# Other span widths in a gated recurrence with a feed-forward layer: 512, 512 and 496 pairs in place of 480, 512 and 512

## The reference, cut to what matters

```python
sig = 1.0 / (1.0 + np.exp(-f_logit))                 # (2, 6080, 256)
f = lower_bound + (1.0 - lower_bound) * sig
for t in range(S):
    h = f[:, t] * h + (1.0 - f[:, t]) * x[:, t]
    y[:, t] = h
h = y.reshape(B * S, D) @ w_in                       # (12160, 256) @ (256, 2048)
g = np.where(h >= 1, h, np.where(h <= -1, 0.0, (h + 1) ** 2 / 4))
return g @ w_out                                     # (12160, 2048) @ (2048, 256)
```

## Time and profile before

| what | us |
| --- | --- |
| median of 3 runs (992.54 to 993.21) | 992.62 |
| the profiled execution | 992.79 |
| its span, first to last instruction | 990.9 |
| TensorE busy | 985.0 (99%) |
| ScalarE busy | 873.6 (88%) |
| VectorE busy | 865.9 (87%) |
| GpSimd busy | 0.2 |
| the chain that ended last | 99% on TensorE |
| granted TensorE clock | 1.00 in all slices |
| DMA | 42.37 MB, 43 GB/s in the mean |

### The profile page before, as it was taken

How to read it: one execution, slowest core, us unless ns; L and a number is a source line. 1 busy time by engine, 2 the same in 40 slices (tenths; PEclk the granted TensorE clock), 3 DMA queues, 4 the chain that set the end, 5 groups by cost and what they waited for, 6 DMA issues and landing times.

```text
span 990.9 us, 12871 instructions
## 1 busy us (share of the span) xinstructions
PE 985.0 (99%) x4366; PEld 817.4 (82%) x4366; DVE 865.9 (87%) x1305; ACT 873.6 (88%) x1543; POOL 0.2 (0%) x4
## 2 busy tenths in 40 slices
PE   9999999999999999999999999999999999999998
PEld 6888888888888888888888888888888888888887
DVE  7998988988988888898888989889888889898775
ACT  8898989989988988998998898899898899898886
POOL 0000000000000000000000000000000000000000
PEclk9999999999999999999999999999999999999999
DMA  7202102101200210210120120021021012000101
GB/s 231 104 1 86 41 1 86 43 1 43 86 1 1 85 43 1 85 43 1 44 85 1 25 88 17 1 83 43 1 83 46 0 42 83 1 1 1 43 1 41
DMA packets 14577, 42.37 MB, mean 43 GB/s; under 512 B 1584, under 2 KB 4912, under 8 KB 14512
## 3 DMA queue, kind: packets, MB, share of 16 engines
q1 hardware_dynamic: 14224, 41.30, 12.2%
q10 hardware_dynamic: 288, 0.26, 0.1%
HBM read 29.10 MB, written 12.45 MB: 42 GB/s over the span
## 4 chain that ended last, share of the span: by engine, by line
PE 99%; DMA 0%; SPq 0%; ACT 0%; issue 0%
PE acc L942 18%; PE acc L943 18%; PE acc L944 18%; PE chain L942 9%; PE chain L943 9%; PE chain L944 9%; PE cross L943 4%; PE cross L942 4%; PE cross L944 4%; PE side L943 2%; PE side L944 2%; PE side L942 2%; DMA w_in_near<-w_in_pairs 0%; PE chain L1103 0%; PE side L1103 0%; PE cross L1103 0%
## 5 line engine op out<-in xcount | busy, mean ns | idle before, releaser
L942 PE MATMUL acc<-g_hi,w_out_lo 128*128 128x512 f32 (+2 forms) x768 | 297.7, 388 | 0.0
L943 PE MATMUL acc<-g_lo,w_out_hi 128*128 128x512 f32 (+2 forms) x768 | 297.3, 387 | 0.0
L944 PE MATMUL acc<-g_hi,w_out_hi 128*128 128x512 f32 (+2 forms) x768 | 297.3, 387 | 0.0
L405 ACT CAST g_hi<-g 128x512 fp32r<-128x512 f32 (+2 forms) x384 | 236.3, 615 | 41.2 <-DVE g L736 35.5
L751 DVE TENSOR_TENSOR g_lo<-g,g_hi 128x512 fp32r<-128x512 f32 (+2 forms) x384 | 262.2, 683 | 9.1 <-ACT g_hi L405 0.5
L398 ACT ACTIVATE g<-g 128x512 f32<-128x512 f32 (+2 forms) x384 | 240.9, 628 | 3.7
L736 DVE SCALAR_TENSOR_TENSOR g<-g,h 128x512 f32<-128x512 f32 (+1 forms) x264 | 180.9, 685 | 46.0 <-ACT g L398 42.7
L380 ACT ACTIVATE g<-h 128x512 f32<-128x512 f32 (+1 forms) x264 | 163.2, 632 | 26.9 <-DVE h L711 24.5
L942 PEld LDWEIGHTS acc<-g_hi,w_out_lo 128*128 128x128 f32 x768 | 144.1, 188 | 30.3 <-DVE g_lo L751 1.2
L944 PEld LDWEIGHTS acc<-g_hi,w_out_hi 128*128 128x128 f32 x768 | 144.2, 188 | 28.5
L943 PEld LDWEIGHTS acc<-g_lo,w_out_hi 128*128 128x128 f32 x768 | 144.2, 188 | 28.2
(11 more groups left out here) (91 smaller groups left out, 955.8 us busy)
## 6 DMA issues: line engine op xcount, KB each, us to landing
gate<-f_logit_chunks SPq DMA_DIRECT2D x18, 512.0 KB, 4.0
y<-x_chunks SPq DMA_DIRECT2D x18, 512.0 KB, 4.0
out_chunks<-result SPq DMA_DIRECT2D x9, 1024.0 KB, 4.2
w_out_f<-w_out_pairs SPq DMA_DIRECT2D x8, 256.0 KB, 4.9
y<-x_chunks SPq DMA_DIRECT2D x4, 496.0 KB, 4.0
gate<-f_logit_chunks SPq DMA_DIRECT2D x4, 496.0 KB, 4.1
w_in_near<-w_in_pairs SPq DMA_DIRECT2D x10, 128.0 KB, 4.4
out_chunks<-result SPq DMA_DIRECT2D x1, 992.0 KB, 4.2
```

Source lines behind the costliest of these rows:

```text
L405: nc.scalar.copy(g_hi[:, t, 0:cols], g[:, t, 0:cols]).then_inc(g_hi_ready[t], 1)
L942: nc.tensor.matmul(dst, w_lo, v_hi, start=start, stop=False, skip_group_check=more)
L943: nc.tensor.matmul(dst, w_hi, v_lo, start=False, stop=False, skip_group_check=more)
L944: return nc.tensor.matmul(dst, w_hi, v_hi, start=False, stop=stop, skip_group_check=more)
```

## The change

Span 0 gets 512 pairs like its neighbours. To keep 3040 pairs in batch 0, spans 8 and 10 get 496 in place of 512. Batch 1 is as before (spans 9 and 11 have 496). All tiles, loads, matmuls and operations follow from `width(q)`.

```diff
-FULL, FIRST_SHORT, LAST_SHORT = 512, 480, 496
+FULL, SHORT = 512, 496
@@
 def width(q):
-    if q == 0:
-        return FIRST_SHORT
-    return LAST_SHORT if q in (SPANS - 1 - BATCH, SPANS - 1) else FULL
+    return SHORT if q >= SPANS - 2 * BATCH else FULL
```

## The result

The changed kernel takes 994.99 us (median of 14 runs, 994.34 to 995.46), the kernel before 992.80 beside it (14 runs): ratio 1.0022, 95% interval 1.0015 to 1.0029. It is slower by 2.2 us, where 991.2 was forecast with a range up to 992.8. The profiled execution has a span of 992.8 us against 990.9.

What follows compares the result with a forecast made beforehand. TensorE, busy 99%, was taken to bound the kernel: matmuls times their step, plus opening and stalls. Terms 3.60 - 4.80 + 0.62 - 0.45 - 0.10 - 0.27 = -1.40 us gave 991.2 from 992.62, range 990.7 to 992.8.

Steps and rivals of the forecast that it cites:

- Preparing the next span: 496-wide windows preparing 496-wide spans (8, 9, 10) stall 0.02 us three times, against 0.32 before: -0.27 us.
- Rival A: First span stays 40 cycles above its columns, so its 512-wide matmuls take 230.0 ns: +1.20 us, 992.4; chance 0.18.
- Rival B: Stalls while preparing the next span stay full, three times 0.32 us: 0.91 above the forecast sum, 992.1; chance 0.14.
- Rival C: First span's 512-wide matmuls hold 236.7 ns because engines and weight loads use memory densely: +3.6 us, 994.8; chance 0.03.
- all cases beyond 2 us slower: Whole kernel slower by over 0.2%, mainly through 236.7 ns matmuls in the first span; chance 0.04.
- 360 x 10.0 = +3.60 for the first span: First span's 360 matmuls go from 480 to 512 columns, 216.7 to 226.7 ns each: +3.60 us.
- -4.80 for spans 8 and 10: 720 matmuls in these spans go from 512 to 496 columns, 226.7 to 220.0 ns each: -4.80 us.
- The stalls of window 3: First span's weight loads waiting for VectorE's g_lo: 0.45 of 0.65 us disappears behind longer matmuls, -0.45 us.
- The 0.22 in window 2: Time lost at the window's start, where the weight load waits for VectorE's g_lo: 13.22 us for 13.00 due.
- the change of spans: At 88 to 106 us, where 480 and 512 columns mix, mixing costs could go: -0.10 us, bounds -0.20 and 0.
- The opening: Before TensorE streams: larger half-loads +0.22, VectorE's drives and scans +0.29, last raw group +0.11; together +0.62 us.

Runs made afterwards that it cites:

- the first experiment: Changed kernel with ScalarE copying u3 ahead of the split of the next span's T1, T2 in windows j = 6: 990.93 us against 992.67, ratio 0.9985.

## Why the prediction was wrong

**The step that failed** is "Preparing the next span". I had found the event, counted that the weight load of p4 would come 0.12 us after its due time, and booked the stall of the one matmul behind it, 0.02 us, three times. It came 0.06 late (the copy ended 2.42 us after the start of p7, not 2.48), and its window lost 0.03 us, once. What I left out is what the late load does to all later matmuls: 25 windows x 0.15. The term was -0.27 and is -0.32 + 3.78 = +3.46. The number was in the trace of before: window 79 ran 0.15 us long over all its 45 matmuls, and I called it the wake of the stall and gave it the length of one window, because in that kernel 512-wide matmuls happened to follow.

**Rival A** held the right state, the offset of 40 cycles in place of 32, and I put it only on the first span. There it did not act, since 512 columns find back by themselves: windows 4 to 6 last 10.88. It would have, had the first span become 496 (10.72 in place of 10.56). I never asked of it what it does to the widths that the change makes more frequent. **Rival B** had three full stalls at 0.91 us; its place was right and its price counted by event, not by what follows. **Rival C** did not occur in the steady windows. Its price was read from rounded times: the three steps from 90.27 to 90.98 are 704 ns together, 234.7 each and not 236.7. The same 233 to 236 ns are seen where 512 columns mix with 480 in window 65 of the version with 480 in span 8, with no DMA transfer beside them. Whether the other engines' work has a part in it was not tested. I gave all cases beyond 2 us slower 0.04; that is where it ended.

**The surer terms.** 360 x 10.0 = +3.60 for the first span is right: 10.88 - 10.40 = 0.48 a window. The slope of 13.3 ns that the Trainium skill gives (TensorE: Matmul & The Clock Gate, Back-to-back issue gap) did not show in the first span, where the measured difference is 10.0; the 480 end of it sits 8 cycles high at both places where it was measured. -4.80 for spans 8 and 10 is right without the late load: 9.90 in the first experiment. The stalls of window 3 went from 0.65 to 11.07 - 10.88 = 0.19, which is -0.46 against -0.45, and the waits of the weight load for g_lo from 1.2 us to this row of the waits of after:

```profile
PEld acc L940 <- DVE g_lo L749: 0.2, 1, 0.2
```

The 0.22 in window 2 stayed (13.82 us for 60 x 0.2267 = 13.60). In the change of spans window 8 still takes 7.09, now for 30 x 226.7 = 6.80, so 0.12 of its excess went; window 9's went from 0.09 to 0.04 (10.17 and 10.24, for 10.08 and 10.20 due). Together that is -0.17 against -0.10.

**The opening** is a small miss. From the first raw matmul to the first 512-wide product it takes 7.85 us against 7.46, +0.39 for my 0.29 + 0.11. But the first raw matmul did not come 0.22 later; it starts at 6.79 here, and at 6.96, 7.29, 6.70, 7.05, 7.11 and 7.04 in the experiments with 512 in the first span, against 7.03 and 6.94 with 480. What 64 KB more ahead of the first weight block cost can't be seen in that spread; nearest to it is nothing. The 7.85 us are 7.81 to 7.85 in four of these six experiments, but 8.35 and 8.51 in two (the first and the one with six wide matmuls); why is open. Without that term the forecast of the sum without a late load is 991.0, and the first experiment measured 990.93.

## What to carry to other kernels

Where one engine streams without a gap, a delay is not worth the time it lasts but the time it takes the stream to find back; so when a trace shows a stretch that runs a few per cent off its step behind a stall, look for what ended it, and ask whether the change takes that away. Price an event by the steps behind it, and look at a steady window's length divided by its instructions, not at busy shares or at idle time: longer steps count as busy, and TensorE's share is 99% with and without the 3.8 us. An operation that a tight wait doesn't need should not stand ahead of the one that it does: putting one cast behind one copy is worth 4 us of 995 here and turns a loss of 2.2 us into a gain of 1.7 (990.93 against 992.67), of which the order alone is some 0.3.

## What the runs showed of the hardware

The step of a stream of three-pass matmuls at the full granted clock, each with its own weight load, in ns and cycles at 2.4 GHz:

| columns | step | above the columns | seen in |
| --- | --- | --- | --- |
| 480 | 216.7 ns, 520 | 40 | first span of before, span 8 of an experiment |
| 496 | 220.0 ns, 528 | 32 | after a 512-wide or 504-wide span |
| 496 | 223.3 ns, 536 | 40 | after a late load, after 480 columns, out of the opening |
| 504 | 226.7 ns, 544 | 40 | spans 8 and 10 of two versions |
| 512 | 226.7 ns, 544 | 32 | every window of 512 alone, also from the second after a late load |

Behind the late load of window 34 the 512-wide stream took 224 to 236 ns a step for nine matmuls and 226 to 227 from then on. Where 512 columns mix with 480 or 504, at the edges of spans, some steps of 512 take 233 to 236 ns as well.

A weight load that was 0.06 us late, its matmul 0.01, brought the 496-wide stream from the one to the other for 260 us; six matmuls of 512 columns brought it back and one did not. What exactly tips it stays open. Three loads 0.06 or 0.07 late with their matmul on time did not, one 0.07 late with its matmul on time did, and in one version a load within 0.01 us of its time did. All of these are at the p4 whose u3 copy ends just when it is due. Open as well are the reason for two steps eight cycles apart, and why 512 columns leave the longer one by themselves and 496 don't.
